# Attention stage of a three-stage kernel: another order of the matmuls and vector steps in each unit, and up to five extra matmuls per unit

## The reference, cut to what matters

```python
for t in range(S):                       # a_re_n, a_im_n: a, scaled to a magnitude of at most 0.999
    new_re = ar * S_re - ai * S_im
    new_im = ar * S_im + ai * S_re
    S_re, S_im = new_re + k_t (x) v_t, new_im
    y[t] = q_t . S_re
x = y, as 3072 rows of 384               # then the two mixtures
```

## Time and profile before

| what | value |
|---|---|
| median of three runs | 2599.39 us |
| the profiled execution | 2598.59 us |
| its span in the profile | 2596.9 us |
| PE busy | 2371.5 us (91%) |
| DVE busy | 1161.4 us (45%) |
| ACT busy | 748.4 us (29%) |
| POOL busy | 188.4 us (7%) |
| mean granted clock of TensorE | 0.933 of full speed |

### The profile page before, as it was taken

One profiled execution on the slowest core, in us unless ns is written; L12 is line 12 of the kernel. 1 busy time (PEld: TensorE's weight loads), 2 busy tenths in 40 slices (PEclk: granted clock), 3 DMA queues, 4 the chain that ended last, 5 costly groups with the idle time before them and its releaser, 6 DMA issues. The chain is left out here.

```text
span 2596.9 us, 41008 instructions
## 1 busy us (share of the span) xinstructions
PE 2371.5 (91%) x14026; PEld 2269.3 (87%) x14027; DVE 1161.4 (45%) x2533; ACT 748.4 (29%) x1293; POOL 188.4 (7%) x176
## 2 busy tenths in 40 slices
PE   0388888899999999999999999999999999599998
PEld 0266767779999999999999999999999999488897
DVE  6777777654443333333333333333333332575543
ACT  4555655342111211112111121111111112244422
POOL 0000000001001001011011011011010000022221
PEclk9876666799999999999999999999999999699999
DMA  3012121101000000000000000000000011344210
GB/s 123 33 34 71 46 70 47 45 23 49 1 25 25 0 25 24 0 24 24 0 24 24 0 24 24 0 24 12 12 24 0 24 43 37 104 148 135 82 36 21
DMA packets 44716, 96.80 MB, mean 37 GB/s; under 512 B 4101, under 2 KB 26651, under 8 KB 44640
## 3 DMA queue, kind: packets, MB, share of 16 engines
q1 hardware_dynamic: 40672, 84.97, 9.5%
q0 software_dynamic: 3968, 10.82, 1.3%
HBM read 161.83 MB, written 10.81 MB: 66 GB/s over the span
## 5 line engine op out<-in xcount | busy, mean ns | idle before, releaser
L984 PE MATMUL bank<-x_parts,w_hi 128*128 (+1 forms) x3072 | 783.7, 336 | 0.1
L869 ACT ACTIVATE h_hi<-bank 128x384 fp32r<-128x384 f32 x512 | 250.2, 492 | 1250.6 <-PE bank L984 1250.5
L984 PEld LDWEIGHTS bank<-x_parts,w_hi 128*128 128x128 f32 x3072 | 554.6, 188 | 0.2 <-DVEq L906 0.2
L938 DVE SCALAR_TENSOR_TENSOR h_lo<-bank,h_hi 128x384 fp32r<-128x384 f32 x512 | 284.2, 557 | 577.4 <-ACT h_hi L869 577.4
L984 PE MATMUL bank<-x_parts,w_lo 128*128 (+1 forms) x1536 | 514.0, 335 | 0.0
L996 PE MATMUL bank<-w_hi,h_hi 128*128 128x384 f32 x1536 | 513.3, 334 | 0.0
L996 PE MATMUL bank<-w_hi,h_lo 128*128 128x384 f32 x1536 | 513.1, 334 | 0.0
L996 PE MATMUL bank<-w_lo,h_hi 128*128 128x384 f32 x1536 | 513.0, 334 | 0.0
L958 DVE SCALAR_TENSOR_TENSOR mixed<-bank,gate,mixed 128x384 f32 (+1 forms) x336 | 207.7, 618 | 442.4 <-PE bank L996 442.4
L984 PEld LDWEIGHTS bank<-x_parts,w_lo 128*128 128x128 f32 x1536 | 289.0, 188 | 0.0
L996 PEld LDWEIGHTS bank<-w_hi,h_lo 128*128 128x128 f32 x1536 | 288.3, 188 | 0.0
(11 more groups left out here) (197 smaller groups left out, 2007.8 us busy)
## 6 DMA issues: line engine op xcount, KB each, us to landing
routed_w_raw<-in_moe_w SPq DMA_DIRECT2D x64, 1536.0 KB, 6.6
w_raw<-in_moe_w SPq DMA_DIRECT2D x32, 768.0 KB, 6.0
q_k<-in_qk SPq DMA_DIRECT2D x24, 512.0 KB, 3.7
decay<-in_a SPq DMA_DIRECT2D x20, 528.0 KB, 5.2
v_rows<-in_v SPq DMA_DIRECT2D x24, 192.0 KB, 2.3
mixed_rows<-mixed SPq DMA_DIRECT2D x4, 1152.0 KB, 4.6
decay<-in_a SPq DMA_DIRECT2D x4, 432.0 KB, 4.8
routed_x<-mixed_rows,gather_now POOLq DMA_INDIRECT x31, 3.6
```

The source lines that it names most:

```text
L869: nc.scalar.activation(h_parts[par][0][:, c, :], h_bank[c], ACT.Relu).then_inc(h_hi, 1)
L938: nc.vector.scalar_tensor_tensor(out=h_parts[par][1][:, c, :], in0=h_bank[c], scalar=0.0, in1=h_parts[par][0][:, c, :].bitcast(F32), op0=A ...
L984: last = nc.tensor.matmul(h_bank[c].rearrange("p (u s) -> p u s", u=SUB), w1_parts[half][w][:, k, c * PT:(c + 1) * PT], mem.x[:, bass.ds(b ...
```

## The change

On **TensorE**, the 8 transposes of k (real and imaginary part together) come first in a unit, ahead of all scores. The odd heads' scores go behind `sum_squares` and `logits`, and four of the `add_to_state` matmuls stand between them. There are extra matmuls, whose results nothing reads: `keep_warm` multiplies the identity by the identity, repeated to 512 columns, in one fp32 matmul. One stands ahead of y in every unit that passes its state on, four behind y in every unit but the last.

On **ScalarE**, both k copies come first, ahead of `guess_inverse`.

On **VectorE**, `invert` comes ahead of `add_squares_of_a`, and the second `scale` instruction comes behind `decay_state`.

```diff
 (VectorE, in the loop over the units)
                 mask(u, 1)
                 product(p, 2)
+                invert(a, 0)
+                sums(p, 2)
+                invert(a, 1)
+                product(p, 3)
                 if p + 1 < UNITS:
                     add_squares_of_a(p + 1)
-                sums(p, 2)
-                product(p, 3)
                 sums(p, 3)
-                invert(a, 0)
+                divide(a)
                 product(p, 4)
-                invert(a, 1)
+                add_state(u)
                 sums(p, 4)
-                divide(a)
+                scale(a, LEFT)
                 product(p, 5)
-                add_state(u)
+                decay_state(u, RE)
                 sums(p, 5)
-                scale(a, LEFT)
+                decay_state(u, IM)
+                product(p, 6)
                 scale(a, RIGHT)
-                product(p, 6)
-                decay_state(u, RE)
                 sums(p, 6)
-                decay_state(u, IM)
                 new_state(u)
 (TensorE)
+            def keep_warm(bank):
+                nc.tensor.matmul(bank[:, :], ident[:, :], ident[:, :].unsqueeze(1).to_broadcast([PT, BANK // PT, PT]),
+                                 start=True, stop=True)
...
                 pe.wait_ge(scaled, 2 * u + 2)
+                if passes_on(u):
+                    for part, bank in enumerate((kt_re, kt_im)):
+                        if kept(u):
+                            pe.wait_ge(k_rows, 2 * kept(u) - 1 + part)
+                        for pair in range(PAIRS):
+                            last = nc.tensor.transpose(pairs(bank)[:, pair, :], qk[:, par, K, part, pair, :], ident[:, :])
+                        last.then_inc(k_back, 1)
                 if u:
                     pe.wait_ge(masked, 2 * u)
                 for h in range(0, H, 2):
                     last = score(h)
                 last.then_inc(scored, 1)
-                if passes_on(u):
-                    turn_k(RE, kt_re)
-                for h in range(1, H, 2):
-                    last = score(h)
-                last.then_inc(scored, 1)
                 if u + 1 < UNITS:
                     sum_squares(u + 1)
-                if passes_on(u):
-                    turn_k(IM, kt_im)
                 if u >= 2:
                     pe.wait_ge(y_copied, u)
                     logits(u - 2)
                 pe.wait_ge(v_landed[u % 3], 16 * (u // 3 + 1))
                 if passes_on(u):
+                    pe.wait_ge(k_rows, 2 * kept(u) + 1)
                     if kept(u):
                         pe.wait_ge(state_read, kept(u))
-                    for part in (RE, IM):
-                        pe.wait_ge(k_rows, 2 * kept(u) + 1 + part)
-                        for h in range(H):
-                            last = add_to_state(part, h)
+                for h in range(1, H, 2):
+                    if passes_on(u):
+                        add_to_state(RE, h - 1)
+                    last = score(h)
+                last.then_inc(scored, 1)
+                if passes_on(u):
+                    pe.wait_ge(k_rows, 2 * kept(u) + 2)
+                    for pair in range(PAIRS):
+                        add_to_state(RE, 2 * pair + 1)
+                        for h in (2 * pair, 2 * pair + 1):
+                            last = add_to_state(IM, h)
                     last.then_inc(kv_done, 1)
                 if u:
                     turn_x(u - 1)
+                if passes_on(u):
+                    keep_warm(kt_re)
...
                 last.then_inc(y_done, 1)
+                if u + 1 < UNITS:
+                    for n in range(4):
+                        keep_warm(sc_a)
```

More of the change, by code:

```diff
@@ L555, in _ @@
                 p = u + NCH + 2
[L556 to L560, removed]
-                if passes_on(u):
-                    place_k_rows(RE, kt_re)
+                if passes_on(u):
+                    for part, bank in enumerate((kt_re, kt_im)):
+                        act.wait_ge(k_back, 2 * kept(u) + part + 1)
+                        if u:
+                            act.wait_ge(y_done, u)
+                        nc.scalar.activation(krow[:, part, :, :], pairs(bank), ACT.Copy).then_inc(k_rows, 1)
                 if u + 1 < UNITS:
                     guess_inverse(u + 1)
-                if passes_on(u):
-                    place_k_rows(IM, kt_im)
                 if u >= 2:
@@ L645, in add_to_state @@
                                             start=True, stop=True)
[L647 to L652, removed]
-                pe.wait_ge(scaled, 2 * u + 2)
+                pe.wait_ge(scaled, 2 * u + 2)
+                if passes_on(u):
+                    for part, bank in enumerate((kt_re, kt_im)):
+                        if kept(u):
[3 more added lines that the diff above has]
+                        last.then_inc(k_back, 1)
                 if u:
```

## The result

The changed kernel takes 2640.75 us (median of four runs, 2634.49 to 2641.08) against 2599.4 us: a ratio of 1.0152, 95% interval 1.0135 to 1.0170. It is 41 us slower. The forecast was 2610 with a range up to 2638: right in its sign, a quarter of the loss in its size.

A forecast was written before the change was run, and what follows sets the result against it. It took a TensorE-ScalarE-VectorE chain to bound the scan units and TensorE the units without scan. Terms 1 + 0 + 2 + 7.7 = +11 us on 2598.59 gave 2609.6, forecast 2610 us, range 2577 to 2638.

The forecast's parts named there:

- the sign: Whole kernel: slower, 2610 us, 0.4% more; the chance of slower was put at 0.57.
- the wait moved from L235 to `mask`: VectorE in scan units: the wait at L235 nearly gone, the long wait now at the second `mask`.
- TensorE idles in mid-unit for 2.4 us: Scan units: TensorE waits some 2.4 us for ScalarE's squares behind the even scores, where before there was no gap.
- `mask` to the end of `scale` takes 9.1 us: VectorE in scan units: second `mask` to end of `scale` grows from 7.3 us to 9.1 us.
- The scan units: 13 units with the scan: mean 22.0 us a unit against 21.9, together +1 us.
- rival 2: Cold spreads: following units lose the clock too, among narrow logits and half-height scores; +40, 2640 us; chance 0.13.
- Units 5/6 and 11/12: Pairs whose first unit waits for the batch's scan: 44 us a pair against 44.0, so 0.
- Units 17/18: TensorE-bound from there: 38 to 42 us against 38.3 before, +2 us.
- Units 19 to 22: Without scan, TensorE's floor decides: 17.7 us each for 15.8, +7.7 us, called the surest term.
- odd scores and four state matmuls 2.3: TensorE between logits and the second `mask` in a warm scan unit: this stretch takes 2.3 us.
- outcome (a): Scan unit with TensorE's clock kept through the sum: 20.2 us; taken for one of eight units.
- the ring: Chain bounding a scan unit: TensorE's scores and sum, ScalarE's guess and squares, then 7.3 us of VectorE; 21.9 us a unit.

The follow-up runs named there:

- fill_squares_wait: The changed kernel with two more extra matmuls behind the even scores, where TensorE waits for the squares: 2625.34 us, ratio 1.0105 to the kernel before.
- four_only: The kernel before with the four extra matmuls behind y and nothing else: 2574.76 us, ratio 0.9870.
- odd_scores_back: The changed kernel with the odd heads' scores put back ahead of the sum of squares, all else kept: 2536.19 us, ratio 0.9738 to the kernel before.
- no_extra: The changed kernel without any extra matmuls, its new orders kept: 2677.47 us, ratio 1.0261 to the kernel before.
- turn_back_behind_sum: The changed kernel without extra matmuls, the imaginary part's four transposes of k put back behind the sum of squares: 2683.73 us, ratio 1.0328 to the kernel before.
- one_behind_sum: The changed kernel's orders with a single extra matmul a unit, right behind the sum of squares: 2662.85 us, ratio 1.0214 to the kernel before.
- square_first_four: The kernel before with `square` first on ScalarE and four extra matmuls behind y: 2535.66 us, ratio 0.9730.
- back_square_first: The changed kernel with odd scores back ahead of the sum, `square` first on ScalarE, VectorE's order of before: 2528.72 us, ratio 0.9731 to the kernel before.

## Why the prediction was wrong, step by step

**Right:** the sign; the wait moved from L235 to `mask`; TensorE idles in mid-unit for 2.4 us (2.48); the sum is cold in those units, `mask` to the end of `scale` takes 9.1 us (9.0: 462.31 to 471.3); a unit with an idle stretch takes 20 to 27 us and its follower opens late and warm; `keep_warm` costs 0.9 us warm (3.67 for four).

**The scan units**, "against 21.9 ... +1 us": the 13 such units took 22.6 us, +9. I gave one of eight the kept clock and three an early recovery; measured, five of the 13 took 25.5 to 25.9 (and unit 0, from a cold start, 28.6), and the four of their followers that are among the 13 took 18.8 to 20.8 for my 17.7. One of these (unit 8) lost the clock behind the logits, which is rival 2's mechanism; units 3, 14 and 16 ran at 1.00 from end to end and took 18.8 to 19.1 even so. The clock fell about the sum in 8 of its 23 units, not in more than half, and in 8 more behind the logits. *Units 5/6 and 11/12* took 46.0 and 48.4 us for 44: +6 for 0. *Units 17/18*: 43.9, +6 for +2.

**Units 19 to 22**, "TensorE's floor decides", "17.7 each", "the surest term": 20.2 each, +17.6 for +7.7. This is the step that failed, and in two ways. The floor itself was too low: unit 20 runs at 1.00 without a gap and takes 18.6 us. And a floor at the warm clock is a bound from below; I took it for the forecast in an order of instructions in which the clock doesn't stay warm (units 19, 21 and 22: 21.7, 20.1 and 20.3 us at 0.84 and 0.92). The four terms are 9 + 6 + 6 + 18 = 39 of the 41 us.

**The mis-sized term** under both sums is "odd scores and four state matmuls 2.3". At 1.00 that stretch takes 3.5 us (564.14 to 567.68), because the two alternate, which I priced at nothing. With it the floor comes to 18.9 for 17.7 (18.6 measured), and outcome (a), the clock kept, to 21.4 for 20.2 (21.2 in units 2, 3 and 8 of fill_squares_wait). By my estimate this one term, 0.9 to 1 us in each of the 20 units that pass a state, is 18 to 20 of the 30 us that I missed.

**Rival 2** named 2640 us and had 0.13. It has the clock lost behind the logits right; its number is in part luck, since it charges the followers' extra time to the clock, and most of them ran at 1.00.

**The attribution was wrong as well.** I charged the loss to the extra matmuls and priced the order at nothing beyond the clock in one place. The runs say the reverse: order of TensorE and ScalarE +2.9%, with VectorE's +2.6%, extra matmuls then -1.1 points, to +1.5%. The sum came out with the right sign from a wrong ledger; it would have advised removing the extra matmuls, and that costs 37 us. My part list left out the question that decides: what the moved odd scores had been covering. In the kernel before they lie between the even scores and the sum, so the squares arrive before TensorE gets there; that cover was 3.7 us and its loss was priced only as "TensorE idles some 2.4 us".

**The sentence from the Trainium skill** ("TensorE: Matmul & The Clock Gate", section "HAM oscillation — how this bites in real kernels"), that idle stretches between bursts drop the clock and closing them keeps it: four_only, fill_squares_wait and odd_scores_back (0.95 over its scan units, 104.6 to 416.9 us, for 0.67 before) agree. By itself it doesn't explain no_extra, where TensorE had no idle time in 47.6 us and a mean clock of 0.57.

**Left open:** which mix of narrow, half-height and full-height matmuls holds the clock without a gap. One guess on it, turn_back_behind_sum, failed; one_behind_sum got the clock back behind the sum, but not for the next transposes and scores. Open too are why the alternation of scores and state matmuls is slow, and why square_first_four and back_square_first end level.

## What to carry to other kernels

Before moving an instruction later, ask what wait it fills where it stands, on its own engine: here eight matmuls moved behind the sum and the logits, and woven between others, cost 100 us: they had covered a 2.4 us wait, they feed the engine that closes the ring, and the weaving made them slower by itself. Price a block of matmuls in the order in which it will run, not by its parts. A floor worked out at an engine's fast clock is no forecast until something shows that the new order holds that clock. And take a change apart before judging its parts: the part that looked like pure cost was the one that gave time back.

## What the runs showed of the hardware

TensorE can be busy without a gap and at a low mean clock: 47.6 of 47.6 us busy at 0.57 in units 21 and 22 of no_extra, and 33.7 of 33.7 us at 1.00 in the same units of odd_scores_back, which differs in the place of eight score matmuls, in their alternation with state matmuls, and in five dense extra ones. A unit is 23.8 us in the one and 16.8 in the other, though the second has 4.4 us more to do at the high clock.

Eight fp32 score matmuls and four state matmuls take 3.5 us in alternation and some 2.0 in one block each, both at a granted clock of 1.00 and without idle time (the changed kernel and odd_scores_back, unit 20).
